# Scores of a chunked linear attention: two heads of a pair on separate partition ranges instead of zero-padded keys

## What is computed

```python
# attention; r, k, v are [4, 8, 768, 48]
for t in range(S):
    kt, vt, rt = (k[:, :, t], v[:, :, t], r[:, :, t])
    cur = np.einsum('bhd,bhe->bhde', u[None] * kt, vt)
    y[:, :, t] = np.einsum('bhd,bhde->bhe', rt, state + cur)
    state = w[None, :, :, None] * state + np.einsum('bhd,bhe->bhde', kt, vt)
...
# then, on x = y laid out as [3072, 384]
h = np.maximum(np.maximum(x @ w1, x @ w2), x @ w3); x = h @ w_out
...
# then the router picks 2 of 8 experts per token
h = np.maximum(x[mask] @ w1[e], 0.0)
out[mask] += top2_w[mask, k, None] * (h @ w2[e])
```

## Time and profile before

| what | us |
|---|---|
| median of 3 runs | 980.56 |
| lowest and highest of them | 980.24 and 982.49 |
| the profiled execution's own time | 977.49 |
| its span, from first to last instruction | 975.6 |
| PE busy in the span | 931.2 |

### The profile page before, as it was taken

One profiled execution on the slowest core, in us unless ns is written; L12 is line 12 of the kernel. 1 busy time (PEld: TensorE's weight loads), 2 busy tenths in 40 slices (PEclk: granted clock), 3 DMA queues, 4 the chain that ended last, 5 costly groups with the idle time before them and its releaser, 6 DMA issues.

```text
span 975.6 us, 18718 instructions
## 1 busy us (share of the span) xinstructions
PE 931.2 (95%) x6410; PEld 926.4 (95%) x6411; DVE 458.3 (47%) x993; ACT 256.2 (26%) x462; POOL 432.1 (44%) x408
## 2 busy tenths in 40 slices
PE   4799999999999999999979989999999999999996
PEld 4699999999999999999969989999999999999996
DVE  7555264636646474654533434253443435252322
ACT  1242221311222131323321431242312224141211
POOL 5445443635444263543533445353443443534343
PEclk9699999999999999999989989999999999999999
DMA  7467211212121121003261331515151525312122
GB/s 174 116 188 226 64 34 59 57 42 55 51 57 40 58 57 32 25 0 93 79 171 42 113 96 57 176 43 183 37 188 56 176 79 174 88 47 69 42 78 64
DMA packets 94959, 85.02 MB, mean 87 GB/s; under 512 B 51994, under 2 KB 84450, under 8 KB 94912
## 3 DMA queue, kind: packets, MB, share of 16 engines
q1 hardware_dynamic: 72816, 53.94, 19.2%
q0 software_dynamic: 12096, 25.69, 8.7%
q10 hardware_dynamic: 10000, 4.82, 1.7%
HBM read 69.55 MB, written 21.15 MB: 93 GB/s over the span
## 4 chain that ended last, share of the span: by engine, by line
PE 44%; DMA 4%; issue 2%; DVE 1%; POOL 1%; POOLq 0%; DVEq 0%; ACT 0%; ACTq 0%; SPq 0%
PE ps L1303 14%; PE ps L1304 14%; PE ps L1305 14%; PE ps L1342 2%; DMA xg<-x_rows,ent_e 1%; DMA prev<-out,ent 1%; DMA out<-yrow,ent 1%; DMA ent<-lists 1%; DMA e_raw<-ew 0%; POOL lists L495 0%; DMA xg<-x_rows,ent 0%; DVE w1l L928 0%; POOL prev L597 0%; POOLq L87 0%; DVE yrow L1020 0%
## 5 line engine op out<-in xcount | busy, mean ns | idle before, releaser
L1303 PE MATMUL ps<-xgh,w1h 128*128 128x256 f32 (+1 forms) x648 | 182.8, 282 | 1.7 <-DVE xgl L994 1.1
L1305 PE MATMUL ps<-xgh,w1l 128*128 128x256 f32 (+1 forms) x648 | 182.8, 282 | 0.0
L1304 PE MATMUL ps<-xgl,w1h 128*128 128x256 f32 (+1 forms) x648 | 182.7, 282 | 0.0
L1303 PE MATMUL ps<-yh,wh 128*128 128x384 f32 x432 | 148.4, 344 | 4.3 <-ACT hmax L1107 1.7
L1197 ACT ACTIVATE gh<-ps 128x512 fp32r<-128x512 f32 x108 | 64.3, 597 | 320.1 <-PE ps L1305 310.5
L1304 PE MATMUL ps<-yl,wh 128*128 128x384 f32 x432 | 145.5, 337 | 0.0
L1305 PE MATMUL ps<-yh,wl 128*128 128x384 f32 x432 | 145.5, 337 | 0.0
L597 POOL DMA_INDIRECT prev<-out,ent x50 | 59.5, 1190 | 188.7 <-DMA ent<-lists 181.1
L1303 PE MATMUL ps<-w2h,gh 128*128 128x384 f32 x408 | 140.1, 343 | 0.3 <-DVE gl L999 0.3
L1304 PE MATMUL ps<-w2l,gh 128*128 128x384 f32 x408 | 137.5, 337 | 0.0
L1305 PE MATMUL ps<-w2h,gl 128*128 128x384 f32 x408 | 137.3, 337 | 0.0
(11 more groups left out here) (172 smaller groups left out, 1688.4 us busy)
## 6 DMA issues: line engine op xcount, KB each, us to landing
ew_raw<-ew SPq DMA_DIRECT2D x28, 768.0 KB, 7.2
v_sb<-vN SPq DMA_DIRECT2D x24, 192.0 KB, 2.6
wraw<-moe_w SPq DMA_DIRECT2D x8, 576.0 KB, 4.8
out<-zrow SPq DMA_DIRECT2D x1, 4608.0 KB, 17.4
x_rows<-x_sb ACTq DMA_DIRECT2D x8, 576.0 KB, 3.5
kn_sb<-kN SPq DMA_DIRECT2D x20, 192.0 KB, 2.7
k_raw<-kT SPq DMA_DIRECT2D x48, 72.0 KB, 1.9
r_raw<-rT SPq DMA_DIRECT2D x48, 72.0 KB, 2.0
```

Source lines behind the costliest of these rows:

```text
L1303: pe.matmul(o, ah, bh, start=start, stop=False)
L1304: pe.matmul(o, ah, bl, start=False, stop=False)
L1305: return pe.matmul(o, al, bh, start=False, stop=stop)
```

## The change

The keys are no longer padded. `k_hat` [128, pair, 128] is the chunk's keys times the table, each pair once, with the first head on partitions 0 to 47 and the second on 64 to 111. Each score matmul reads its head's 48 partitions of `k_hat` and of `q_hat`; the first heads of all pairs write bank 3, the second heads bank 4, and the calls alternate between the two. In the built program these matmuls are tiles of 64 by 128 in PE's array, at row 0 and at row 64; all others are 128 by 128. Both `s_mm` signals now come at the end (after the seventh and the eighth matmul), the mask works on a head of all pairs instead of two pairs with both heads, and `outputs` waits for both masks at its start. The table `wk` is written by one DVE instruction and need not be cleared.

```diff
@@ tables
-            own(pool.memset(wk[:, :, :, :], 0.0))
...
-            pool.sem_inc(wk_clear, 1)
...
-            dve.wait_ge(wk_clear, 1)
-            for h, rows in enumerate(HALF):
-                dve.tensor_tensor(wk[rows, :, h, :], wkn[rows, :, :], along(CH, 3)[rows], ALU.mult).then_inc(tab_ok, 1)
             own.settle()
+            dve.tensor_tensor(wk[:, :, :], wkn[:, :, :], along(CH, 3), ALU.mult).then_inc(tab_ok, 1)
             dve.tensor_tensor(wq[:, :, :], wq[:, :, :], along(CH, 2), ALU.mult).then_inc(tab_ok, 1)
-            dve.wait_ge(tab_ok, 2)
+            dve.wait_ge(tab_ok, 1)
             dve.tensor_tensor(wkn[:, :, :], wkn[:, :, :], along(CH, 4), ALU.mult).then_inc(tab_ok, 1)
@@ keys, on POOL
-                pool.tensor_tensor(k_pad[:, :, :, :], k_raw[:, c, :, :].rearrange("d q (a j) -> d q a j", a=1).to_broadcast([P, PAIRS, 2, CH]),
-                                   wk[:, :, :, :], ALU.mult).then_inc(kpad_ok, 1)
+                pool.tensor_tensor(k_hat[:, :, :], k_raw[:, c, :, :], wk[:, :, :], ALU.mult).then_inc(khat_ok, 1)
@@ masks, on DVE
-                    dve.tensor_tensor(scores[:, 2 * n:2 * n + 2, :, :].rearrange("j q h i -> j (q h) i"),
+                    dve.tensor_tensor(scores[:, :, n, :],
@@ products, on PE
                 for p in range(PAIRS):
                     for h in range(2):
-                        n = 2 * (p % 2) + h
-                        mm = pe.matmul(ps[3 + p // 2][:, n * CH:(n + 1) * CH], k_pad[:, p, h, :], q_hat[cc % 2][:, p, :], start=True, stop=True)
-                    if p % 2:
-                        mm.then_inc(s_mm, 1)
+                        rows = slice(h * HB, h * HB + HD)
+                        mm = pe.matmul(ps[3 + h][:, p * CH:(p + 1) * CH], k_hat[rows, p, :], q_hat[cc % 2][rows, p, :], start=True, stop=True)
+                        if p == PAIRS - 1:
+                            mm.then_inc(s_mm, 1)
@@ outputs, on PE
-                    if p % 2 == 0:
-                        pe.wait_ge(mask_ok, 2 * g + p // 2 + 1)
+                    if p == 0:
+                        pe.wait_ge(mask_ok, 2 * g + 2)
```

More of the change, by code:

```diff
@@ L116, in build @@
         wq = sb("wq", [P, PAIRS, CH], where=turn1)
-        wk = sb("wk", [P, PAIRS, 2, CH], where=turn1)
+        wk = sb("wk", [P, PAIRS, CH], where=turn1)
         wkn = sb("wkn", [P, PAIRS, CH], where=turn1)
@@ L123, in build @@
         v_sb = sb("v_sb", [P, BS, PAIRS, PD], where=turn1)
-        k_pad = sb("k_pad", [P, PAIRS, 2, CH], where=turn1)
+        k_hat = sb("k_hat", [P, PAIRS, CH], where=turn1)
         q_hat = [sb(f"q_hat{i}", [P, PAIRS, CH], where=turn1) for i in range(2)]
@@ L199, in build @@
         const_ok = sem("const_ok")
-        wk_clear, tab_ok = sem("wk_clear"), sem("tab_ok")
+        tab_ok = sem("tab_ok")
         nat_mm, nat_ok = sem("nat_mm"), sem("nat_ok")
@@ L204, in build @@
         v_in = [sem(f"v_in{i}") for i in range(BS)]
-        kpad_ok, kupd_ok = sem("kpad_ok"), sem("kupd_ok")
+        khat_ok, kupd_ok = sem("khat_ok"), sem("kupd_ok")
         q_ok, rk_ok, rku_ok = sem("q_ok"), sem("rk_ok"), sem("rku_ok")
@@ L279, in load_turned @@
                 else:
-                    sp.wait_ge(kpad_ok, g - BS + 1)
+                    sp.wait_ge(khat_ok, g - BS + 1)
                     sp.wait_ge(q_ok, g - BS + 1)
@@ L520, in _ @@
             pool.wait_ge(w_in, 32)
-            pool.wait_ge(tab_ok, 2)
+            pool.wait_ge(tab_ok, 1)
             keys(0, 0)
@@ L651, in _ @@
             own(dve.tensor_tensor(last_n, last, up, ALU.mult))
-            dve.wait_ge(wk_clear, 1)
-            for h, rows in enumerate(HALF):
-                dve.tensor_tensor(wk[rows, :, h, :], wkn[rows, :, :], along(CH, 3)[rows], ALU.mult).then_inc(tab_ok, 1)
             own.settle()
+            dve.tensor_tensor(wk[:, :, :], wkn[:, :, :], along(CH, 3), ALU.mult).then_inc(tab_ok, 1)
             dve.tensor_tensor(wq[:, :, :], wq[:, :, :], along(CH, 2), ALU.mult).then_inc(tab_ok, 1)
-            dve.wait_ge(tab_ok, 2)
+            dve.wait_ge(tab_ok, 1)
             dve.tensor_tensor(wkn[:, :, :], wkn[:, :, :], along(CH, 4), ALU.mult).then_inc(tab_ok, 1)
-            dve.wait_ge(tab_ok, 4)
+            dve.wait_ge(tab_ok, 3)
             def queries(b, cc):
@@ L1240, in _ @@
             pe.wait_ge(const_ok, 1)
-            pe.wait_ge(tab_ok, 4)
+            pe.wait_ge(tab_ok, 3)
             for p in range(PAIRS):
@@ L1247, in products @@
                 c, g = cc % BS, chunk(b, cc)
-                pe.wait_ge(kpad_ok, g + 1)
+                pe.wait_ge(khat_ok, g + 1)
                 pe.wait_ge(q_ok, g + 1)
```

## The result

The changed kernel took 967.89 us (median of 4 runs, 965.49 to 971.5), the kernel before 980.40 us beside it (4 runs, 979.41 to 982.49): a ratio of 0.9881, with a 95% interval from 0.9852 to 0.991. That is 0.9 us from the 967 forecast. The time agrees better than its terms do: one was too small, one too large, one did not show at all, and a cost was missing.

A forecast was written before the change was run, and what follows sets the result against it. PE's passes were taken to bound the periods, and a chain over POOL, DVE and PE the prologue. Savings of 1.9 + 9.7 + 1.8 = 13.4 us from the 980.56 median gave 967, range 959 to 979.

The forecast's parts named there:

- Part 1: Prologue path to `q_hat`: one table instruction and a shorter POOL key product save 1.9 us, bounds 0.7 and 2.8.
- Part 2: Score passes in the periods: two heads overlap, 9 steps for 16, less two form changes; 0.46 us a call, 9.7 in all.
- Part 3: Three prologue calls: faster score passes save 0.9 us in chunk 0, 0 in chunk 1, 0.9 in chunk 2; 1.8 in all.
- Rival 3: Prologue clock rises later, so the outputs from 40.6 on take twice as long: 3 us more, 970; chance 0.07.
- Part 4: Late signals and masks are covered by the update's matmuls: worth 0, or 0.5 us once or twice in the prologue.
- the named check: Sign of error: PE's waits for `hmax` growing above 1.4 us, since hidden blocks then lie closer together.
- Rival 1: Score passes: the heads' weight loads go one after the other, nothing overlaps and nothing is lost; 977 to 980, chance 0.20.
- rival 2: Score calls: form changes cost 0.16 to 0.36 us each and the heads don't overlap; slower, 986 to 995, chance 0.16.

The follow-up runs named there:

- before, tiles alone: The kernel before with padded keys, wide POOL product and two `wk` instructions kept; only score matmuls, banks, signals and masks as in the change: 971.9 us, ratio 0.9952.
- changed, entries later: The changed kernel with POOL's indirect DMAs of a period's entries moved from the period's start to behind the third `hidden_low`: 969.13 us, ratio 0.9903.
- the last run: The kernel before with both score signals for the masks raised at the end of the products, nothing else changed: 976.61 us in one run.

## Why the prediction was right, and where it was not

**What bounds the kernel.** Right: in the periods PE's passes are the time. The calls' 11.2 us would have arrived whole but for 3.1 us of stalls and 1.4 us of clock.

**Part 1, forecast 1.9, measured 0.8 at `q_hat`.** The step "on the path to `q_hat` this leaves 0.70 for the table and 1.19 for the shorter block" was right in its terms: one `wk` of 0.69 us instead of 1.40, and `wkn` 1.75 instead of 2.83, 1.08 less. What failed is "The clearing of `wk` and its wait are off this path". The clearing stood ahead of POOL's other clears, and taking it away put them beside DVE's copy, which cost 1.1 us at the head of the same chain: `wk` begins at 9.78 instead of 8.70. So `q_hat` begins at 12.78 and not at 11.7. I had looked at what waited for the removed instruction, not at what moved up into its place.

**Part 2, forecast 9.7, measured 11.2.** The overlap is as forecast, and both terms are close. The steps: I counted 9, with b1 going beside a2; it is 8, since b1 goes beside a1 and b2 beside a2, 7 ns behind. That saves 0.89 us a call instead of 0.78. The changes of form: 0.094 more ahead of the first score pass, 0.10 in the first step, 0.09 more from the last score pass to the first transpose, and 0.055 in the first transpose's step, 0.34 together for the 0.32 of the sum. That is the 0.16 that I took between 0 and 0.36, and the run with more changes gives 0.18 each. Together 0.54 us a call instead of 0.46. The size is right, but not its reason: I took the 0.16 for the end of a matmul with the next weight load hidden behind it. In the kernel before, the first score pass's weight load starts 0.17 us ahead of that pass (which is at 120.07), beside the last `hidden` pass; in the changed one the loads stand idle for 0.25 us, and the first starts 2 ns ahead of its pass. The loads, before and changed:

```profile
119.90 0.36 PEld L1255 LDWEIGHTS ps<-q_hat,k_pad 128*128 128x128 f32 x2
```

```profile
120.70 0.19 PEld L1250 LDWEIGHTS ps<-q_hat,k_hat 48*128 48x128 f32 x2 [0.25 <-issue]
```

The same holds at the first transpose, 0.11 us ahead there and 2 ns here. So the load is not hidden at a change of form, and that the price came out as taken is luck. The Trainium skill, TensorEngine Tiling (Array Packing), Key Properties, has both halves of this, parallel tiles and a drain at a change of mode. The trace agrees with the first by the 7 ns, and with the second in so far as the weight load no longer runs ahead and a change costs 0.17 us; the first tile pass starts 0.27 us behind a `hidden` pass of 0.34, by its modelled end not quite behind it.

**Part 3, forecast 1.8, measured none.** The prologue ended 1.0 us later in the first profile and 0.7 in the second, though it began its scores 0.7 earlier. The sum took the rates of the earlier trace rows as given; they are not. Rival 3 had named the clock of the prologue, with 3 us and a chance of 0.07. PE's timeline of the first profile, 13 to 48:

```profile
13.91 2.08 PE L1250 MATMUL ps<-q_hat,k_hat 48*128 48x128 f32 x16
...
18.48 3.54 PE L1285 MATMUL ps<-v_sb,scores 128*128 128x48 f32 x16
...
47.23 0.66 PE L1298 MATMUL ps<-yh,wh 128*128 128x384 f32 x1 [1.22 <-issue]
```

Chunk 0's outputs take 3.54 us, as at half rate (the PEclk of a window says nothing before the clock's first recorded change: for this stretch it reads 1.00). Those of before took 1.91, behind scores in the full form for 2.92 us, with the rate rising on the way:

```profile
18.82 1.91 PE L1290 MATMUL ps<-v_sb,scores 128*128 128x48 f32 x16
```

From 42 on the outputs of chunk 2 are at half rate again, where the earlier trace rows have them at the full one, and the window says so:

```profile
40.00:50.30 10.30, 8.28 (x40) 7.77 (x40) 6.17 (x9) 2.93 (x4) 3.87 (x13) 0.57 0.34 88
```

In the second profile chunk 0's outputs and chunk 1's scores were at full rate, and the time was lost from 28 to 47 instead. So the sum's rates did not hold. More than this one pair of profiles can't say, as all eleven profiles without unread matmuls show:

| kernel | score matmuls | first score pass | chunk 0's outputs take | prologue ends |
|---|---|---|---|---|
| before | full | 14.59 | 1.91 | 46.20 |
| changed, full form | full | 13.74 | 1.91 | 47.79 |
| before, late signals | full | 14.59 | 1.91 | 49.24 |
| before, tiles alone | tiles | 14.72 | 1.91 | 48.98 |
| changed | tiles | 13.91 | 3.54 | 47.23 |
| changed, second profile | tiles | 13.89 | 1.91 | 46.92 |
| changed, copy as maximum | tiles | 12.73 | 3.54 | 44.37 |
| changed, entries later | tiles | 13.88 | 3.54 | 47.20 |
| changed, one head | tiles | 13.89 | 3.54 | 48.87 |
| changed, head by head | tiles | 13.89 | 3.54 | 51.95 |
| changed, more changes of form | tiles | 15.33 | 3.54 | 55.45 |

The three kernels with full-form scores alone end their prologues up to 3.0 us apart, so neither a loss of 1.0 us nor a gain of 1.8 can be read from one profile of each. What is shown is that this part did not arrive where it could be seen, and that the clock moves the prologue's end by more than this part was meant to gain. That chunk 0's outputs ran at full rate behind full-form scores in three profiles of three, and behind tiles in two of eight, points to rival 3's reason, that the short passes let the clock stay low there. It is not shown: two profiles of one kernel differ in this too.

**Part 4, forecast 0.** The late signals cost nothing in the calls by the last run. The new stalls of 3.1 us are not in any term, and the named check, PE's waits for `hmax`, did not catch them.

**The sum.** Forecast −13.4: −1.9, −9.7, −1.8, 0. Read from the first profile: −0.7 at the first scores, but with it a prologue of +1.0 in all; calls −11.2; stalls +3.1; clock at 95 us +1.4; the rest −0.9; together −6.6, and the spans say −6.5. The medians say −12.5, so the runs without a profile had more than the first profile shows; the second one has −10.3 in its span. That the forecast hit the median to 0.9 us is luck in part: by the profile, part 2 gave 1.5 us more than its term, the stalls and the clock at 95 us took back 4.5, parts 1 and 3 did not arrive in the prologue, and the spread of the runs covers the difference. Rival 1 is excluded by 1.09 us where it needed 1.7, rival 2 by the overlap.

## What to carry to other kernels

Where PE sets the time and a matmul contracts over at most half of the partitions, put its partner on the other half, issue the two one behind the other into two banks, and price it by steps: two passes side by side cost one step, each change of form some 0.17 us, so do many pairs between two changes and don't interleave them with full matmuls. When you remove an instruction, list what moves up into its place on its queue and what it then runs beside. In a prologue full of gaps take rates from no single profile; a few unread matmuls in its gaps were worth nearly as much here (9.8 to 11.2 us) as the whole change, though by the profiles only 3.4 to 3.7 us of it in the prologue itself.

## What the runs showed of the hardware that I had not expected

- Two fp32 matmuls on disjoint rows start each of their passes 7 ns apart, with weight loads overlapping as well; the second is free (8 passes alone take 1.09 us, 16 take 1.09 us).
- The same matmuls ordered head by head take 1.64 us: adjacency in the order decides, though three passes coincide with others near the change of heads even so.
- A change between the 128-row and the 48-row form costs 0.17 to 0.18 us, and it is spread over both sides: a later first pass, a long first step of 0.21 us, a longer way to the next form. The first weight load starts 2 ns ahead of its pass there, and 0.17 us ahead between full forms.
- A DVE copy of 128x4 waited 1.0 us for a row of POOL clears, and one by maximum (0.13 us) didn't wait at all.
- Around POOL's indirect DMAs PE stood still for up to 0.9 us and DVE for up to 3.8 with nothing shown that they wait for, in some sessions and hardly in others.
